# Stacking the short third tile of a Fourier transform into one product, and reordering the work of its last image

## What is computed

```python
def phi(x):
    proj = np.einsum('bhsd,df->bhsf', x, w_phi)
    proj = proj - np.max(np.abs(proj), axis=-1, keepdims=True)
    return np.concatenate([np.exp(proj), np.exp(-proj)], axis=-1)
q_p, k_p = (phi(q), phi(k))
kv = np.einsum('bhsf,bhsd->bhfd', k_p, v)
z = np.sum(k_p, axis=2)
num = np.einsum('bhsf,bhfd->bhsd', q_p, kv)
den = np.einsum('bhsf,bhf->bhs', q_p, z)[..., None] + 1e-06
x = num / den                              # heads side by side
...
mixed = np.real(np.fft.fft(np.fft.fft(x, axis=1), axis=2))
u = x + mixed
un = (u - mean(u)) / np.sqrt(var(u) + 1e-06)
x = u + np.maximum(un @ w_ch1, 0.0) @ w_ch2
...                                        # once more: norm, gain, two products, residual
```

## Time and profile before

| | |
|---|---|
| median of 3 runs | 1003.7 us (1002.39 to 1004.59) |
| the profiled execution | 1002.03 us |
| its span | 1000.2 us |
| PE busy | 992.2 us, 99% |
| DVE busy | 653.0 us, 65% |
| ACT busy | 557.3 us, 56% |
| POOL busy | 364.8 us, 36% |
| matmuls of step A (L661) | 168 |
| granted clock of TensorE | 1.00 over the span |

### The profile page before, as it was taken

One profiled execution on the slowest core, in us unless ns is written; L12 is line 12 of the kernel. 1 busy time (PEld: TensorE's weight loads), 2 busy tenths in 40 slices (PEclk: granted clock), 3 DMA queues, 4 the chain that ended last, 5 costly groups with the idle time before them and its releaser, 6 DMA issues.

```text
span 1000.2 us, 16743 instructions
## 1 busy us (share of the span) xinstructions
PE 992.2 (99%) x5866; PEld 918.7 (92%) x5866; DVE 653.0 (65%) x1156; ACT 557.3 (56%) x1018; POOL 364.8 (36%) x362
## 2 busy tenths in 40 slices
PE   9999999998999999999999999999999999999998
PEld 8999999998999989989999899998999999989997
DVE  6676769889966568465684656755577555765443
ACT  5655555755665565555555666556655666634341
POOL 4633234443443263331732317224172232621210
PEclk9999999999999999999999999999999999999999
DMA  6333131301252312323223231232324322242202
GB/s 183 73 93 86 44 73 39 70 13 34 80 162 75 106 46 93 87 73 106 64 74 104 61 100 64 74 106 64 95 64 138 106 67 92 64 130 81 64 1 64
DMA packets 101312, 80.29 MB, mean 80 GB/s; under 512 B 56944, under 2 KB 81776, under 8 KB 101232
## 3 DMA queue, kind: packets, MB, share of 16 engines
q1 hardware_dynamic: 100992, 78.91, 28.1%
q10 hardware_dynamic: 240, 0.33, 0.1%
HBM read 66.10 MB, written 4.72 MB: 71 GB/s over the span
## 4 chain that ended last, share of the span: by engine, by line
PE 95%; DVE 3%; issue 1%; SPq 0%; DMA 0%; ACT 0%; DVEq 0%; ACTq 0%
PE bank L1176 39%; PE bank L1153 35%; PE bank L409 6%; PE bank L422 5%; PE bank L375 3%; PE bank L661 2%; PE bank L681 2%; PE bank L393 1%; PE bank L427 1%; PE bank L369 1%; DVE xall L545 1%; DMA rawqk_second<-qkT 0%; PE bank L351 0%; SPq L559 0%; DVE xall L538 0%
## 5 line engine op out<-in xcount | busy, mean ns | idle before, releaser
L1176 PE MATMUL bank<-w2op,hid 128*128 128x512 f32 x1728 | 423.3, 390 | 0.0
L1176 PEld LDWEIGHTS bank<-w2op,hid 128*128 128x128 f32 x1728 | 321.6, 188 | 53.4 <-issue 0.3
L1153 PE MATMUL bank<-x_T,w1op 128*128 128x384 f32 x1152 | 208.1, 335 | 0.0
L1153 PEld LDWEIGHTS bank<-x_T,w1op 128*128 128x128 f32 x1152 | 201.2, 188 | 3.9
L1153 PE MATMUL bank<-x_B,w1op 128*128 128x384 f32 x864 | 173.5, 336 | 0.0
L1153 PEld LDWEIGHTS bank<-x_B,w1op 128*128 128x128 f32 x864 | 154.4, 188 | 11.4
L1347 POOL TENSOR_TENSOR w_sums<-st_w 128x256 f32<-128x256 f32 x48 | 49.5, 1032 | 224.2 <-DVE w1op L1383 224.2
L1463 DVE SCALAR_TENSOR_TENSOR hid<-part_s,hid 128x384 fp32r<-128x384 f32 x141 | 98.2, 723 | 37.7 <-ACT hid L1459 37.5
L1315 POOL TENSOR_TENSOR x_sums<-xraw 128x256 f32<-128x256 f32 x30 | 22.3, 765 | 194.4 <-ACT xraw L1268 124.3
L1404 DVE TENSOR_TENSOR w2op<-st_w,w2op 128x1024 fp32r<-128x1024 f32 x48 | 62.8, 1308 | 45.9 <-ACT w2op L1400 45.9
L1459 ACT ACTIVATE hid<-part_s 128x384 fp32r<-128x384 f32 x141 | 73.3, 524 | 31.1 <-DVE part_s L1433 31.1
(11 more groups left out here) (181 smaller groups left out, 1500.5 us busy)
## 6 DMA issues: line engine op xcount, KB each, us to landing
st_w<-w1a SPq DMA_DIRECT2D x24, 512.0 KB, 3.5
st_w<-w2a SPq DMA_DIRECT2D x24, 512.0 KB, 3.7
st_w<-w1b SPq DMA_DIRECT2D x24, 512.0 KB, 3.4
st_w<-w2b SPq DMA_DIRECT2D x24, 512.0 KB, 3.6
v<-v SPq DMA_DIRECT2D x16, 256.0 KB, 3.9
out<-xall SPq DMA_DIRECT2D x16, 256.0 KB, 2.1
rawqk<-qkT SPq DMA_DIRECT2D x14, 288.0 KB, 4.1
rawqk<-qkT SPq DMA_DIRECT2D x14, 256.0 KB, 3.6
```

The lines of the kernel that those rows point to most:

```text
L1153: last = nc.tensor.matmul(dst, w1op[g % 2][:, a, W1OP.index(w), c, :], xop[x][:, b, c, :], start=name in ("M2", "M1", "M7") and k_ == 0, s ...
L1176: last = nc.tensor.matmul(acc[t0 + t][:, :], hid[name, g % 2][:, x, P * t:P * (t + 1)], w2op[g % 2][:, y, j, :], start=first and k_ == 0, ...
```

## The change

The third tile's three products become one. In the rows of the third tile that held zeros, the rounded operand and the rounded constant now hold more: rows 0 to 31 the rounded part (as before), rows 32 to 63 the rounded operand again, against the remainder of the constant, and rows 96 to 127 the remainder of the operand, against the rounded constant. One matmul over 128 rows then sums all three. The extra row moves from row 32 to row 64 (`XROW`); its constant is exact, but in the C products its remainder still has to be added, by one matmul over rows 64 to 95 alone. Second, in the tail two divisions come before the folds, four operations move from VectorE to GpSimd, and ScalarE rounds B21 and B11 earlier.

```diff
@@ -78,7 +79,15 @@
-    return {"cs": rows(np.concatenate([cs, odd]), HT), "ss": rows(ss, HT), "cd": rows(cd, 2),
+    def stacked(a, extra=None):
+        out = np.concatenate([rows(a[:2 * P], 2), np.zeros((P, 1, a.shape[1]), np.float32)], axis=1)
+        for q_ in (0, 1, 3):
+            out[T2 * q_:T2 * (q_ + 1), 2] = a[2 * P:]
+        if extra is not None:
+            out[XROW, 2] = extra
+        return f(out)
+
+    return {"cs": stacked(cs, odd[0]), "ss": stacked(ss), "cd": rows(cd, 2),
             "sd": rows(sd, 2), "alt": rows(alt, 1)[:, 0]}
@@ -454,6 +464,14 @@
+    def dve_stack_const(dve):
+        dve.wait_ge(s_split_lo, 2)
+        rows = slice(T2, 2 * T2)
+        for n in ("cs", "ss"):
+            nc.vector.tensor_tensor(cst[n, "hi"][rows, 2, :], raw[n][rows, 2, :], f32(cst[n, "hi"][rows, 2, :]),
+                                    ALU.subtract).then_inc(s_stack, 1)
     UNITS = ((0, 1, 2), (3, 4, 2))
@@ -643,22 +661,28 @@
         if name[0] == "S":
-            pe.wait_ge(oo_hi, 2 * b + h + 1)
+            pe.wait_ge(oo_hi, 2 * (2 * b + h + 1))
             pe.wait_ge(oo_lo, 2 * b + h + 1)
             pe.wait_ge(s_zero, 4)
-        else:
-            pe.wait_ge(ee_hi, 2 * b + h + 1)
+            pe.wait_ge(s_stack, 2)
+        else:
+            pe.wait_ge(ee_hi, 2 * (2 * b + h + 1))
             pe.wait_ge(ee_lo, 2 * b + h + 1)
...
         if name == "CX":
-            steps = [(ee_both[:, :, t, HD], cst["cs", y][:, t, :]) for t in range(HT) for y in ("hi", "lo")]
-        else:
-            steps = [(src[x][:, t, c0:c1], cst[mat, y][:, t, :]) for t in range(HT) for x, y in HL_]
-        for k_, (lhsT, rhs) in enumerate(steps):
-            last = nc.tensor.matmul(dst, lhsT, rhs, start=k_ == 0, stop=k_ == len(steps) - 1)
+            steps = [(dst, ee_both[:, :, t, HD], cst["cs", y][:, t, :]) for t in range(2) for y in ("hi", "lo")]
+            c0, c1, dst = HD, HD + 1, dst[0:1, :]
+        else:
+            steps = [(dst, src[x][:, t, c0:c1], cst[mat, y][:, t, :]) for t in range(2) for x, y in HL_]
+        steps.append((dst, src["hi"][:, 2, c0:c1], cst[mat, "hi"][:, 2, :]))
+        if name[0] == "C":
+            rows = slice(XROW, XROW + T2)
+            steps.append((dst, src["lo"][rows, 2, c0:c1], cst["cs", "hi"][rows, 2, :]))
+        for k_, (to, lhsT, rhs) in enumerate(steps):
+            last = nc.tensor.matmul(to, lhsT, rhs, start=k_ == 0, stop=k_ == len(steps) - 1)
         last.then_inc(a_done, 1)
@@ -691,10 +715,10 @@
                 src = xall[0:1, g_, b, :].rearrange("p (q c) -> p q c", c=P)[:, 0:4:3, :]
-                dst = xall[T2:T2 + 1, 4 + g_, b, :].rearrange("p (q c) -> p q c", c=P)[:, 0:4:3, :]
+                dst = xall[XROW:XROW + 1, 4 + g_, b, :].rearrange("p (q c) -> p q c", c=P)[:, 0:4:3, :]
             else:
                 src = xall[0:1, g_, b, P:3 * P]
-                dst = xall[T2:T2 + 1, 4 + g_, b, P:3 * P]
+                dst = xall[XROW:XROW + 1, 4 + g_, b, P:3 * P]
             nc.scalar.activation(dst, src, ACT.Copy, scale=sc).then_inc(s_exrow, 1)
@@ -750,21 +774,29 @@
             act.wait_ge(oo_done, 2 * b + h + 1)
-            nc.scalar.copy(folded(oo, "hi", h), oo_raw[:, :, 1 - h:P]).then_inc(oo_hi, 1)
+            which, src, ready = oo, oo_raw[:, :, 1 - h:P], oo_hi
         else:
             act.wait_ge(ee_done, 2 * (2 * b + h + 1))
-            nc.scalar.copy(folded(ee, "hi", h), ee_raw[:, :, 0:P + h]).then_inc(ee_hi, 1)
+            which, src, ready = ee, ee_raw[:, :, 0:P + h], ee_hi
+        nc.scalar.copy(folded(which, "hi", h), src).then_inc(ready, 1)
+        act.wait_ge(ready, 2 * (2 * b + h) + 1)
+        nc.scalar.copy(folded(which, "hi", h)[T2:2 * T2, 2, :], src[0:T2, 2, :]).then_inc(ready, 1)
 
...
         if odd:
-            dve.wait_ge(oo_hi, 2 * b + h + 1)
-            nc.vector.tensor_tensor(folded(oo, "lo", h), oo_raw[:, :, 1 - h:P], f32(folded(oo, "hi", h)),
-                                    ALU.subtract).then_inc(oo_lo, 1)
-        else:
-            dve.wait_ge(ee_hi, 2 * b + h + 1)
-            nc.vector.tensor_tensor(folded(ee, "lo", h), ee_raw[:, :, 0:P + h], f32(folded(ee, "hi", h)),
-                                    ALU.subtract).then_inc(ee_lo, 1)
+            dve.wait_ge(oo_hi, 2 * (2 * b + h + 1))
+            which, src, ready = oo, oo_raw[:, :, 1 - h:P], oo_lo
+        else:
+            dve.wait_ge(ee_hi, 2 * (2 * b + h + 1))
+            which, src, ready = ee, ee_raw[:, :, 0:P + h], ee_lo
+        hi, lo = folded(which, "hi", h), folded(which, "lo", h)
+        nc.vector.tensor_tensor(lo[:, 0:2, :], src[:, 0:2, :], f32(hi[:, 0:2, :]), ALU.subtract)
+        if not odd:
+            rows = slice(XROW, XROW + T2)
+            nc.vector.tensor_tensor(lo[rows, 2, :], src[rows, 2, :], f32(hi[rows, 2, :]), ALU.subtract)
+        nc.vector.tensor_tensor(hi[3 * T2:P, 2, :], src[0:T2, 2, :], f32(hi[0:T2, 2, :]), ALU.subtract)\
+            .then_inc(ready, 1)
@@ -958,6 +990,8 @@
         dve_features(dve, g, 0)
+        if g == 3:
+            dve_stack_const(dve)
         if g == STAT_SLOT:
@@ -1320,21 +1354,21 @@
-    def dve_first_sum(dve, name, a, c):
+    def first_sum(eng, unit, name, a, c):
...
-            dve.wait_ge(xt_cp, BT)
+            eng.wait_ge(xt_cp, BT)
...
-            dve.wait_ge(w1_sum, 4)
-            dve.wait_ge(w1_hi, 3)
-            dve.wait_ge(w1_lo, 3)
+            eng.wait_ge(w1_sum, 4)
+            eng.wait_ge(w1_hi, 3)
+            eng.wait_ge(w1_lo, 3)
...
-            dve.wait_ge(unit_done, 5 * PAIRS)
-            dve.wait_ge(x_sum, 3)
-        else:
-            dve.wait_ge(tr_done, ROUNDS * (PAIRS - 1))
-            dve.wait_ge(x_sum, 9)
-        nc.vector.tensor_tensor(xsum(name, 0), a, c, ALU.subtract).then_inc(x_sum, 3)
+            eng.wait_ge(unit_done, 5 * PAIRS)
+            eng.wait_ge(x_sum, 6)
+        else:
+            eng.wait_ge(tr_done, ROUNDS * (PAIRS - 1))
+            eng.wait_ge(x_sum, 9)
+        unit.tensor_tensor(xsum(name, 0), a, c, ALU.subtract).then_inc(x_sum, 3)
@@ -1731,6 +1765,7 @@
                     pool.wait_ge(s_split_hi, 5)
+                    pool.wait_ge(s_stack, 2)
                     nc.gpsimd.memset(f32(tx[:, :]), 0.0)
@@ -1738,8 +1773,12 @@
             mix_F_high(pool, nc.gpsimd, B - 2)
+            first_sum(pool, nc.gpsimd, "T2", xblock("B22"), xsum("T1", 0))
+            first_sum(pool, nc.gpsimd, "T4", xblock("B21"), xsum("T2"))
             mix_G_low(pool, nc.gpsimd, B - 2)
             mix_G_high(pool, nc.gpsimd, B - 2)
+            x_lo_sum(pool, nc.gpsimd, 0, "T2")
+            x_lo_sum(pool, nc.gpsimd, 0, "T3")
             mix_F_low(pool, nc.gpsimd, B - 1)
@@ -1777,13 +1816,13 @@
             act_fold_hi(act, B - 1, 0, False)
+            act_x_hi(act, 0, 0)
+            act_x_hi(act, 0, 1)
             for r in range(ROUNDS):
...
             act_place288(act, B - 2)
-            act_x_hi(act, 0, 0)
             act_kv_copy(act, l, 0)
             act_kv_copy(act, l, 1)
-            act_x_hi(act, 0, 1)
             act_x_hi(act, 0, 2)
@@ -1840,15 +1879,11 @@
             dve_finish(dve, l - 1, 0)
+            dve_finish(dve, l - 1, 1)
             dve_fold_lo(dve, B - 1, 0, True)
             dve_fold_lo(dve, B - 1, 0, False)
-            dve_first_sum(dve, "T2", xblock("B22"), xsum("T1", 0))
-            dve_finish(dve, l - 1, 1)
-            dve_first_sum(dve, "T4", xblock("B21"), xsum("T2"))
             x_lo_block(dve, nc.vector, 0, "B21")
             x_lo_block(dve, nc.vector, 0, "B11")
-            x_lo_sum(dve, nc.vector, 0, "T2")
-            x_lo_sum(dve, nc.vector, 0, "T3")
             dve_finish(dve, l, 0)
```

6 lines of the change are left out of this document (4 added, 2 removed).

## The result

The changed kernel takes 1009.79 us (median of 4 runs, 1009.26 to 1010.83) against 1003.22 us before (4 runs, 1002.39 to 1004.59): ratio 1.0065, 95% interval 1.0052 to 1.0078. The forecast was 1005.8 with a range up to 1009.0, so the direction was right and the size too small, beyond the range. The profiled execution took 1010.83 us around a span of 1008.9.

The account below looks back on a forecast made before the run. TensorE, busy 99% of the span, was taken as the bound. Slots (-2.4 + 1.2 + 0.6 = -0.6 us) and tail (+3.2) gave +2.6, put on 1003.2: 1005.8 us, range 1000.0 to 1009.0.

Parts of the forecast that it names:

- the mechanism of the tail: Tail: GpSimd and VectorE alternate on SBUF operations, six of GpSimd's precede B11's remainder; second layer 3.2 us late.
- the K·V wait: Last K·V product: its 0.69 us wait for VectorE's division goes, since both divisions come first.
- Rivals 1 and 2: Tail: queue short enough, reordering pays, 1000.1 us, 25%; or pieces without waits pass as one, 1002.7 us, 17%.
- the price of that idling: Before S1: some 5 us of TensorE idling instead of 2.16, with no clock cost in the sum.
- Range and chances: Forecast's section on spread: a clock fall behind S1 carries only the upper end; faster 0.28, same 0.26, slower 0.46.
- the base of the sum: Whole kernel: the average of four executions before the change, 1003.2 us, to which the sum was added.
- the product over 32 rows: C0, C1, CX: twelve added products over partitions 64 to 95, seven exposed at 0.09 us each, 0.6 us.
- nearest row: C0's first to second matmul, a change between fp32 and rounded operands: 0.22 us instead of 0.133, so 0.09 per product.
- slots 9 and 13: K·V product there waits for the late division: loses 0.2 us instead of gaining 0.4, twice, 1.2 us.
- the constants' stacking at nothing: Slot 3: two subtractions in VectorE's idle time; GpSimd's work some 3 us later but still in time; no cost.
- in case the cover was thin: Slot 4: if the idle time doesn't cover the constants' subtractions, VectorE's fold is late first; no size given.
- Rival 3: Each 32-row product empties the array: seven exposed at 0.70 us cost 4.9 instead of 0.6; 1010.1 us, 8%.

Follow-up runs that it names:

- experiment 4: The changed kernel with one wait added: GpSimd starts T2 only when VectorE's remainders of the last image's first half are done; 1007.63 us.
- Experiment 3: Filler matmuls keep TensorE busy where it idled; here the changed kernel with 32 of them between M1 and S1 of the last image: 1009.21 us.
- experiment 5: The kernel before with only S0 and S1 stacked, GpSimd stacking the constant in slot 2: 1003.51 us with the old tail, 1001.49 us with a new one.

## Why the prediction was right or wrong

**Right: the mechanism of the tail, in its sizes.** That all six of GpSimd's operations pass before B11's remainder is what the timelines show: last divisions 2.7 late (2.5 forecast), S1 3.2 late (6.02 less 2.85; 2.8 forecast), the K·V wait gone, 4.70 us of idling ("some 5 us"). Rivals 1 and 2 needed fewer turns and fall with the same rows. That it is GpSimd's queue that stretches VectorE's pieces is shown by experiment 4: with GpSimd waiting they last 0.28 and 0.42.

**Wrong: the price of that idling.** The tail was forecast 3.2 us late and is 5.8. The first step that failed is the one in "Range and chances" that left the clock out of the sum: "TensorE idled 2.16 us at the full grant of 1.00" was read off one trace as what 2.16 us do, and only the upper end of the range got the rest. S1's seven matmuls at 0.24 instead of 0.133 are 0.75 us more, and the twelve of M6 and M7 take 3.84 (255.35 to 259.19) instead of 2.2, together 2.4; the two matmuls saved in S1 give 0.3 back, and C1 is 5.3 us late instead of 3.2. Experiment 3 tells how much of it is the clock's. With the filler, at the full clock, the second layer is still 4.3 us late: C1 is 3.9 late, since it waits for VectorE's even half, and 0.4 is lost behind it. So of the missing 2.6 us the clock is 1.5, and 1.1 is VectorE's later work, a term that was sized too small. The same idling in a second trace of the same kernel had the clock at 0.50. In 51 of 78 runs it fell, so the base of the sum, 1003.2, was itself a mean over two groups whose means lie 2 us apart.

**Wrong: the product over 32 rows.** Taken at 0.09 us from the change between fp32 and rounded operands; measured 0.4 for C0's in slot 4, and about 0.25 each for C1's and CX's in slot 6, which follow each other. The bounds (0 and 0.70) held it, but the "nearest row" was not near. Slot 4 came out at +0.07 instead of -0.31, slots 6 and 10 at -0.02 instead of -0.22. The Trainium skill's rule that I had set beside it, "TensorE: Matmul & The Clock Gate", section Why this matters for your kernels, says that a lone matmul over 32 rows takes the time of one over 128. In this trace it doesn't: its record lasts 0.39 us and theirs 0.30. In the run with 64 rows only the first of three, the one behind the change, lasts 0.40, the other two 0.29. So what one pays are the changes around it, of which the rule says nothing.

**Right in kind, short in size: slots 9 and 13.** The wait for the division is there (0.30 us before K·V at 127.06), but each costs 0.46 instead of 0.2. It is VectorE's chain that sets it, not the product over 32 rows: with full rows TensorE comes earlier, waits 0.68 us, and loses the same 0.45.

**Wrong: the constants' stacking at nothing.** It stood in VectorE's idle time, as said, but GpSimd waits for it, and that wait has a queue behind it. GpSimd and VectorE of after:

```profile
41.19 0.34 POOL L1769 MEMSET tx<- 128x290 f32 x1 [4.90 <-DVE ss_hi L472]
...
47.45 1.35 POOL L733 TENSOR_TENSOR EH<-xall 128x384 f32<-128x384 f32 x1
```

```profile
48.84 0.56 DVE L760 TENSOR_TENSOR ee_raw<-EL,EH 128x381 f32<-128x381 f32 x1 [0.91 <-POOL EH L733]
```

The fold of slot 4 waits 0.91 us for GpSimd's sums, the divisions behind it are late, and the next K·V product starts 0.26 later: the order of events that the forecast named in case the cover was thin. Two other kernels bear it out: where GpSimd stacks the constant itself (experiment 5) slot 3 loses 0.01 us, and in the one with full rows, where GpSimd clears another tile behind the same wait (0.31 us), slot 3 loses 0.51. In slot 14 another 0.25 us goes to the transposes of the norm, which start later behind VectorE (L1148 at 208.31); the rest of slot 14's miss was not followed up. The misses add up: 0.38 in slot 4, 0.2 each in 6 and 10, 0.26 each in 8 and 12, 0.26 in 3, 0.66 in 14, and 0.07 each in 9 and 13 are 2.3, so the slots are +1.7 instead of -0.6.

Rival 3 had nearly the right time (1010.1), but by luck: its seven exposed products over 32 rows cost 1.9 us by these prices, and 1.6 by the slots of the kernel with full rows, not 4.9; the clock, the slots' waits and VectorE's later work made up the rest.

## What to carry to other kernels

A stretch in which TensorE waits is priced by what follows it too: look at the clock in several executions of the same kernel before calling one trace its state, and if an edit makes such a wait longer, add the matmuls behind it at twice their pitch, as an upper bound: where another engine is late too, less is lost (2.4 us by the pitch, 1.5 by the filler here). Operations of 32 partitions or 128 columns are not small while GpSimd has a queue on SBUF tiles: count operations on both engines, not elements, and give GpSimd only what can run beside VectorE's work on PSUM. A product over fewer rows is only worth it if the change of rows, here 0.2 us each way, is paid less often than a matmul of 0.13 us is saved.
